# One head's scores as an fp32r product of stacked half terms, in the later batches of an attention and MLP kernel

## The chip, the cores and the metric

The kernel runs on one core of a Trainium2 chip. The metric is the device time of one execution in microseconds (us), from runs of the same program; lower is better.

## What is computed

The reference is a gated linear attention followed by a two-stage MLP. Cut to what matters:

```python
# q, k, v, o_gate: (4, 8, 768, 40); i_gate, f_gate: (4, 8, 768), all fp32
for t in range(S):
    m_new = maximum(f_gate[:, :, t] + m, i_gate[:, :, t])
    f_stab = exp(f_gate[:, :, t] + m - m_new); i_stab = exp(i_gate[:, :, t] - m_new); m = m_new
    C = f_stab * C + i_stab * outer(v_t, k_t)        # per batch and head, 40 x 40
    n = f_stab * n + i_stab * k_t
    y[:, :, t] = sigmoid(o_t) * (C @ q_t) / max(|n . q_t|, 1)
x = y as (4, 768, 320)
u = x + (relu(x.T @ w_tok1) @ w_tok2).T              # over the 768 tokens
out = u + relu(u @ w_ch1) @ w_ch2                    # over the 320 channels, 1536 hidden
```

## The kernel before

Time is cut into six chunks of 128 tokens. Within a chunk the recurrence becomes products: for each head the 128x128 scores k·q are multiplied by a matrix of decays and then applied to the values; the state of the chunks before enters by one more product. The eight heads go in three groups of 3, 3 and 2 heads (`HEADS`), so that a batch has 6 x 3 = 18 steps (`STEPS`). Step m belongs to chunk c = m // 3 and group g = m % 3. The program is written out by hand, one in-order list for each engine, with semaphores between them; nothing is scheduled by a planner.

**Where the attention of a batch runs.** Batch 0 has nothing beside it. The attention of batch b + 1 is spread over the MLP of batch b: its last stage has 24 slots (`SLOTS`), and in each slot every engine also does one place of `attention(b + 1, m)`. In batch 0 slot s holds place s - 3, in batches 1 and 2 slot s holds place s + 2, and places 0 and 1 stand in the stages before (`step_in`). A slot of the MLP is `hidden(slot)`, eight fp32r products of 384 columns on TensorE (lines 1222 to 1227); then `Relu` into `h_hi` on ScalarE (L755) and the remainder `h_lo` on VectorE (L974); then `project(slot)`, nine fp32r products of 320 columns (L1151). TensorE's order is hidden(s), the attention's place, project(s - 1).

**One place of the attention, for batches 1 to 3.** In the order of each engine:
- TensorE: the scores of step m (`step_scores`, L1063) into the one bank `pS`; the state's product (L1075); the values of step m - 2 (L1099, L1120).
- VectorE: `scores` (L851, `pS` times the decays in `gb`, which sets `p_ready`), `state` (L881, L890), `p_low` (L860), and in the places with g = 1 the five operations of `values` (L901 to L912).
- ScalarE: three exponentials of the next step (`exps`, L613), `p_high` (L623, waits for `p_ready`), in the places with g = 2 also `chunk_start` (L595, L599) and `x_high` (L647), in those with g = 0 `v_middle` (L603). With g = 2 the exponentials stand behind `p_high`.
- GpSimd: `rest` (L489, L491), `mask` (L499), and once a chunk `weigh` (L517), L551, L556, `scale_q` (L507) and `x_low` (L521).

**The score product.** The keys of a group, 3 heads x 40 rows, are the stationary operand `kd` (120 rows, 128 columns). The queries are in `qz`, in which each head has 128 columns of its own and zeros in the rows of the other heads, so that one fp32 product of 384 columns (256 in group 2) gives the scores of all heads of the group. `qz` is zeroed once, and three DMAs for each chunk fill the rows that are not zero.

**What the DMA queue does.** Nearly all loads stand in one list on SyncE. In it `load_chunk` for a chunk is `load_scores` (`kd`, `qz`), `load_decays` (`gb`), `load_values` (`kv`), `load_inter` (`gq`, `qd`). The two chunks (1, 0) and (1, 1) are followed by `load_o(1)`, the output gates of batch 1 into `x`, for which `sigmoid` on ScalarE waits in slot 1 of batch 0 (slot 0 in later batches). A wait in this list holds all that stands behind it.

## Time and profile before

| | us |
|---|---|
| median of 3 runs | 459.25 (458.14 to 460.07) |
| the profiled execution's own time | 460.83 |
| its span in the profile | 459.1 |
| TensorE busy | 440.7 (96%) |
| VectorE busy | 259.1 (56%) |
| ScalarE busy | 209.4 (46%) |
| GpSimd busy | 209.1 (46%) |
| chain that ended last, TensorE's share | 83% |

The profile is of one execution. A busy share is an average over stages with different limits, so that a change in one stage is judged by that stage's own rows. Names are PE for TensorE (PEld its weight loads), DVE for VectorE, ACT for ScalarE, POOL for GpSimd, SP for SyncE. Records of one engine overlap at their ends: the time that one operation takes from its engine is the distance from its start to the next start, a little less than its duration. An fp32 product shows as two records.

### The profile page before, as it was taken

Reading aid. Unit: us, or ns where it says so; the run is one execution under the profiler, and the core shown is the slowest. Engines: PE = TensorE matmul, PEld = TensorE weight load, DVE = VectorE, ACT = ScalarE, POOL = GpSimd, SP = SyncE. Lnnn points to the kernel's source line nnn. Section 1 sums busy time; section 2 is a strip of 40 time slices with the busy share of each in tenths; the row PEclk is TensorE's granted clock in tenths of the full one; section 3 lists DMA queues with packets and bytes.
Section 4 is the critical chain, followed back from the end, with each engine's and each line's share of the span. In section 5 each row is a group of like instructions: output and inputs, shape, how many; then the busy total and the mean of one; then the engine's idle time right before and its main releaser. Section 6 shows DMA issues by size and latency. Waiting matters only on the chain.

```text
span 459.1 us, 9511 instructions
## 1 busy us (share of the span) xinstructions
PE 440.7 (96%) x3463; PEld 407.9 (89%) x3463; DVE 259.1 (56%) x592; ACT 209.4 (46%) x517; POOL 209.1 (46%) x293
## 2 busy tenths in 40 slices
PE   7899989998999998999999998999999998999996
PEld 3587878998999997999999997899999997999996
DVE  8588965678865346776663236677674326222212
ACT  3665449665555247655552136755552213211120
POOL 7524410888886242988871204698883000000000
PEclk9899999999999999999999999999999999999999
DMA  7666991343344414544344013444410010000101
GB/s 215 191 172 192 348 256 39 104 115 129 95 134 136 140 44 115 148 127 131 127 152 141 1 44 87 144 135 140 126 60 1 1 43 1 0 2 0 45 1 43
DMA packets 36617, 47.38 MB, mean 103 GB/s; under 512 B 3357, under 2 KB 29083, under 8 KB 36571
## 3 DMA queue, kind: packets, MB, share of 16 engines
q1 hardware_dynamic: 35674, 45.76, 33.1%
q10 hardware_dynamic: 896, 1.02, 0.6%
q8 instruction: 28, 0.46, 0.4%
q14 instruction: 19, 0.15, 0.1%
HBM read 42.73 MB, written 4.03 MB: 102 GB/s over the span
## 4 chain that ended last, share of the span: by engine, by line
PE 83%; issue 6%; DVE 4%; ACT 3%; POOL 2%; DMA 1%; ACTq 0%; DVEq 0%; POOLq 0%
PE pC L1151 32%; PE pA L1222 7%; PE pA L1223 7%; PE pA L1224 7%; PE pS L1063 6%; PE pA L1151 5%; PE pY L1120 4%; PE pA L1226 3%; PE pA L1227 3%; PE pY L1099 2%; PE pN L1075 2%; DMA x<-o_gate_dram 1%; PE pA L1181 1%; POOL vw L517 1%; DVE pb L860 1%
## 5 line engine op out<-in xcount | busy, mean ns | idle before, releaser
L974 DVE SCALAR_TENSOR_TENSOR h_lo<-pA,h_hi 128x384 fp32r<-128x384 f32 x96 | 53.5, 557 | 148.0 <-ACT h_hi L755 147.9
L755 ACT ACTIVATE h_hi<-pA 128x384 fp32r<-128x384 f32 x96 | 46.9, 489 | 138.7 <-PE pA L1227 138.6
L1151 PE MATMUL pC<-wc_hi,h_hi 128*128 128x320 f32 x288 | 94.1, 327 | 0.8 <-DVE wc_lo L841 0.8
L1151 PE MATMUL pC<-wc_lo,h_hi 128*128 128x320 f32 x288 | 88.7, 308 | 0.0
L1151 PE MATMUL pC<-wc_hi,h_lo 128*128 128x320 f32 x288 | 88.5, 307 | 0.0
L489 POOL TENSOR_TENSOR gb<-gb,pb 128x384 f32<-128x384 f32 (+1 forms) x54 | 51.7, 957 | 65.7 <-ACT pb L623 65.4
L1222 PE MATMUL pA<-uT_hi,wc_hi 128*128 128x384 f32 x192 | 65.3, 340 | 1.9 <-DVE uT_hi L952 1.9
L1223 PE MATMUL pA<-uT_lo,wc_hi 128*128 128x384 f32 x192 | 64.7, 337 | 0.0
L1224 PE MATMUL pA<-uT_hi,wc_lo 128*128 128x384 f32 x192 | 64.3, 335 | 0.0
L1151 PEld LDWEIGHTS pC<-wc_hi,h_hi 128*128 128x128 f32 x288 | 54.0, 188 | 2.1 <-DVE h_lo L974 1.1
L1151 PEld LDWEIGHTS pC<-wc_lo,h_hi 128*128 128x128 f32 x288 | 54.2, 188 | 0.1
L1151 PEld LDWEIGHTS pC<-wc_hi,h_lo 128*128 128x128 f32 x288 | 54.0, 188 | 0.0
L613 ACT ACTIVATE gb<-gb,aT 128x128 f32<-128x128 f32 x144 | 47.6, 392 | 1.5 <-POOL gb L499 1.5
L1063 PE MATMUL pS<-qz,kd 120*128 120x384 f32 (+1 forms) x126 | 47.1, 454 | 0.0
L623 ACT ACTIVATE pb<-gb 128x384 bf16<-128x384 f32 (+1 forms) x54 | 26.4, 489 | 36.0 <-DVE gb L851 35.5
L860 DVE TENSOR_TENSOR pb<-gb,pb 128x384 bf16<-128x384 f32 (+1 forms) x54 | 38.6, 716 | 0.1
L1222 PEld LDWEIGHTS pA<-uT_hi,wc_hi 128*128 128x128 f32 x192 | 36.0, 187 | 3.0 <-DVE uT_hi L952 2.9
L521 POOL TENSOR_TENSOR x_lo<-x,x_hi 128x320 fp32r<-128x320 f32 x24 | 21.5, 896 | 33.4 <-ACT x_hi L647 33.4
L1224 PEld LDWEIGHTS pA<-uT_hi,wc_lo 128*128 128x128 f32 x192 | 36.0, 188 | 0.0
L1223 PEld LDWEIGHTS pA<-uT_lo,wc_hi 128*128 128x128 f32 x192 | 36.0, 188 | 0.0
L499 POOL TENSOR_SCALAR_AFFINE_SELECT gb<-gb 128x384 f32<-128x384 f32 (+1 forms) x54 | 29.8, 581 | 5.9 <-DMA gb<-g_dram 5.9
L851 DVE TENSOR_TENSOR gb<-pS,gb 128x384 f32<-128x384 f32 (+1 forms) x63 | 31.8, 504 | 1.1 <-PE pS L1063 0.8
(128 smaller groups left out, 885.0 us busy)
## 6 DMA issues: line engine op xcount, KB each, us to landing
gb<-g_dram SPq DMA_DIRECT2D x18, 512.0 KB, 4.0
kv<-kvN_dram SPq DMA_DIRECT2D x24, 324.0 KB, 4.1
kd<-kT_dram SPq DMA_DIRECT2D x24, 180.0 KB
qz<-qT_dram SPq DMA_DIRECT2D x72, 60.0 KB
out_dram<-u SPq DMA_DIRECT2D x24, 160.0 KB, 1.9
qd<-qT_dram SPq DMA_DIRECT2D x20, 180.0 KB, 2.6
gq<-g_dram SPq DMA_DIRECT2D x45, 60.0 KB
wc_raw<-w_ch_dram SPq DMA_DIRECT2D x6, 384.0 KB, 5.8
```

What stands on the lines that cost most here:

```text
L489: nc.gpsimd.tensor_tensor(tile, tile, pb[:, g, 0, 0:HEADS[g], :], ALU.subtract).then_inc(p_rest, 1)
L499: nc.gpsimd.affine_select(out=tile, in_=tile, compare_op=ALU.is_ge, fill=NEG, base=0, pattern=[[0, HEADS[g]], [1, L]], channel_multiplier= ...
L613: last = nc.scalar.activation(tile, tile, ACT.Exp, bias=aT[:, c, bass.ds(head, 1)])
L755: nc.scalar.activation(h2[0][:, slot % 2], pA[slot % 2][:, 0:HALF], ACT.Relu).then_inc(h2_hi, 1)
L851: nc.vector.tensor_tensor(tile, scores_bank(ba, m)[:, 0:n * L].rearrange("p (h t) -> p h t", h=n), tile, ALU.mult).then_inc(p_ready, 1)
L860: nc.vector.tensor_tensor(pb[:, g, 2, 0:n, :], gb[:, c % Q, GH * g:GH * g + n, :], pb[:, g, 1, 0:n, :], ALU.subtract).then_inc(p_split, 1)
L974: nc.vector.scalar_tensor_tensor(h2[1][:, slot % 2], pA[slot % 2][:, 0:HALF], 0.0, h2[0][:, slot % 2].bitcast(F32), ALU.max, ALU.subtract) ...
L1063: mm(scores_bank(ba, m)[:, 0:n * L], kd[0:n * D, r, g, :], qz[0:n * D, r, g, 0:n, :].rearrange("p h t -> p (h t)"), start=True, stop=True) ...
L1151: ins = mm(dst, a[p], b[q], start=first and n == 0, stop=last and n == 2)
L1222: mm(dst, wc1[0][:, t, f], uh[:, t, cols], start=t == 0, stop=False)
L1223: mm(dst, wc1[0][:, t, f], ul[:, t, cols], start=False, stop=False)
L1224: mm(dst, wc1[1][:, t, f], uh[:, t, cols], start=False, stop=False)
```

## The change

Batch 0 keeps the product above. From batch 1 on each head has an fp32r product of 128 columns of its own, three (or two) in a step. Both operands have 120 rows in which the 40 dimensions stand three times: rows 0 to 39 pair the keys' high half with the queries' remainder, rows 64 to 103 the keys' remainder with the queries' high half, and the other 40 rows the two high halves. So one pass sums three terms. The host lays the rows out in a new array `kq`.

The halves are made on the chip for every step: a load of 120 rows x 768 values into `kq_raw`; a copy to fp32r of the whole tile into `kq_stack` (`step_high`, ScalarE); two subtractions over 40 rows x 384 on VectorE (`step_low`), one for the keys, one for the queries, each on its rows alone. They stand at the end of place m for step m + 1 (places 2 to 5), for both m + 1 and m + 2 in place 6, and for m + 2 later; the last places make the first three steps of the next batch. The first three steps of batch 1 are made by GpSimd (`prepare_first`). `gq` has two buffers in place of three for the later batches, and `load_values` stands ahead of `load_decays`.

```diff
+FIRST_PREPARED = 3
+PREPARES_AT = 2
+TWO_AT = 6
+K_LOW, Q_LOW = slice(64, 64 + D), slice(0, D)
...
+        def prepares(ba, m):
+            if m < PREPARES_AT:
+                return []
+            steps = [m + 1] if m < TWO_AT else [m + 1, m + 2] if m == TWO_AT else [m + 2]
+            n = STEPS + (FIRST_PREPARED if ba < B - 1 else 0)
+            return [later(ba, k) for k in steps if k < n and later(ba, k) >= FIRST_PREPARED]
...
+            def load_step(ba, m):
+                c, g = divmod(m, NG)
+                k = later(ba, m)
+                if k < NG:
+                    sp.wait_ge(s_mm, STEPS)
+                elif k < NG + FIRST_PREPARED:
+                    sp.wait_ge(kq_first, 2 * (k - NG + 1))
+                else:
+                    sp.wait_ge(kq_lo, 2 * (k - NG - FIRST_PREPARED + 1))
+                sp.dma_start(kq_raw[:, g], kq[ba - 1, c, :, g]).then_inc(kq_in[g], 16)
...
             def load_rest(ba, c):
-                if ba > 0:
-                    load_decays(ba, c)
                 load_values(ba, c)
+                load_decays(ba, c)
+                load_step(ba, NG * c + 2)
                 if c > 0:
-                    load_inter(ba, c)
+                    load_query_decays(ba, c)
+                    load_queries(ba, c)
             def load_chunk(ba, c):
-                load_scores(ba, c)
+                load_two_steps(ba, c)
                 load_rest(ba, c)
...
+            def prepare_first(m):
+                _, g = divmod(m, NG)
+                pool.wait_ge(kq_in[g], 16)
+                raw, stack = step_tiles(kq_raw, g), step_tiles(kq_stack, g)
+                nc.gpsimd.tensor_copy(kq_stack[:, g, :, 0:HEADS[g], :], kq_raw[:, g, :, 0:HEADS[g], :]).then_inc(kq_first_hi, 1)
+                pool.wait_ge(kq_first_hi, m + 1)
...
+                    if n == NC:
+                        for m in range(FIRST_PREPARED):
+                            prepare_first(m)
                     pool.wait_ge(v_hi, n - NC + 1)
...
                 if ba > 0 and m % NG == 0 and 0 <= m < STEPS:
                     v_middle(ba, m // NG)
+                for k in prepares(ba, m):
+                    step_high(k)
                 c = chunk_at(ba, m, 1)
                 if c is not None:
                     x_high(ba, c)
+            def step_high(k):
+                g = k % NG
+                act.wait_ge(kq_in[g], 16 * (k // NG + 1))
+                act.wait_ge(s_mm, STEPS + k - NG + 1)
+                nc.scalar.activation(kq_stack[:, g, :, 0:HEADS[g], :], kq_raw[:, g, :, 0:HEADS[g], :],
+                                     ACT.Copy).then_inc(kq_hi, 1)
...
+                if ba > 0:
+                    for k in prepares(ba, m):
+                        step_low(k)
                 c = chunk_at(ba, m, 0)
                 if c is not None and (ba > 0 or c > 0):
                     values(ba, c)
+            def step_low(k):
+                raw, stack = step_tiles(kq_raw, k % NG), step_tiles(kq_stack, k % NG)
+                dve.wait_ge(kq_hi, k - FIRST_PREPARED + 1)
+                nc.vector.tensor_tensor(stack[0][K_LOW], raw[0][K_LOW], stack[0][K_LOW].bitcast(F32),
+                                        ALU.subtract).then_inc(kq_lo, 1)
+                nc.vector.tensor_tensor(stack[1][Q_LOW], raw[1][Q_LOW], stack[1][Q_LOW].bitcast(F32),
+                                        ALU.subtract).then_inc(kq_lo, 1)
...
+                pe.wait_ge(p_ready, STEPS + k)
+                for j in range(HEADS[g]):
+                    last = mm(scores_bank(ba, m)[:, j * L:(j + 1) * L], kq_stack[:, g, 0, j, :], kq_stack[:, g, 1, j, :],
+                              start=True, stop=True)
+                last.then_inc(s_mm, 1)
```

How the lists of the engines change, at three places. First VectorE, from the values of a chunk (end of a place with g = 1) through the place with g = 2. Before:

```order
L909 RECIPROCAL den<-den 128x8 [waits y_den]
L912 TENSOR_TENSOR x<-x,den 128x320 [waits y_read,y_den]
L974 SCALAR_TENSOR_TENSOR h_lo<-pA,h_hi 128x384 [waits h2_hi]
L851 TENSOR_TENSOR gb<-pS,gb 128x256 [waits e_exp,s_mm]
L881 TENSOR_TENSOR stn<-pN,blocks 120x123 [waits st_added,y_mm,n_mm]
L890 SCALAR_TENSOR_TENSOR st<-st,gq,stn 120x123 [waits n_read,st_added,gq_exp]
L860 TENSOR_TENSOR pb<-gb,pb 128x384 [waits p_mid]
L974 SCALAR_TENSOR_TENSOR h_lo<-pA,h_hi 128x384 [waits h2_hi]
```

And now:

```order
L1006 RECIPROCAL den<-den 128x8 [waits y_den]
L1009 TENSOR_TENSOR x<-x,den 128x320 [waits y_read,y_den]
L1084 SCALAR_TENSOR_TENSOR h_lo<-pA,h_hi 128x384 [waits h2_hi]
L948 TENSOR_TENSOR gb<-pS,gb 128x256 [waits e_exp,s_mm]
L978 TENSOR_TENSOR stn<-pN,blocks 120x123 [waits st_added,y_mm,n_mm]
L987 SCALAR_TENSOR_TENSOR st<-st,gq,stn 120x123 [waits n_read,st_added,gq_exp]
L957 TENSOR_TENSOR pb<-gb,pb 128x384 [waits p_mid]
L1031 TENSOR_TENSOR kq_stack<-kq_raw,kq_stack 40x384 [waits kq_hi]
L1033 TENSOR_TENSOR kq_stack<-kq_raw,kq_stack 40x384
L1084 SCALAR_TENSOR_TENSOR h_lo<-pA,h_hi 128x384 [waits h2_hi]
```

Two subtractions, which wait for ScalarE's `kq_hi`, stand ahead of the next slot's `h_lo`. In the place with g = 1 they stand ahead of the values too. Second, ScalarE in a place with g = 2 and the one with g = 0 behind it, before and now:

```order
L595 ACTIVATE gq<-gq 120x384 [waits gq_in2]
L599 ACTIVATE vb<-kv 128x328 [waits y_mm,kv_in1]
L647 ACTIVATE x_hi<-x 128x320 [waits h1_mm,x_ready]
L755 ACTIVATE h_hi<-pA 128x384 [waits c2_mm,c1_mm]
L613 ACTIVATE gb<-gb,aT 128x128 [waits g_masked]
L613 ACTIVATE gb<-gb,aT 128x128 x2
L623 ACTIVATE pb<-gb 128x384 [waits y_mm,p_ready]
L603 ACTIVATE vb<-kv 128x328 [waits v_rest]
L755 ACTIVATE h_hi<-pA 128x384 [waits c2_mm,c1_mm]
```

```order
L686 ACTIVATE vb<-kv 128x328 [waits y_mm,kv_in1]
L736 ACTIVATE kq_stack<-kq_raw 120x768 [waits s_mm,kq_in1]
L744 ACTIVATE x_hi<-x 128x320 [waits h1_mm,x_ready]
L852 ACTIVATE h_hi<-pA 128x384 [waits c2_mm,c1_mm]
L700 ACTIVATE gb<-gb,aT 128x128 [waits g_masked]
L700 ACTIVATE gb<-gb,aT 128x128 x2
L710 ACTIVATE pb<-gb 128x384 [waits y_mm,p_ready]
L690 ACTIVATE vb<-kv 128x328 [waits v_rest]
L736 ACTIVATE kq_stack<-kq_raw 120x2x256 [waits s_mm,kq_in2]
L852 ACTIVATE h_hi<-pA 128x384 [waits c2_mm,c1_mm]
```

The copy comes behind everything that its place had, apart from `x_hi`. Third, SyncE's list from chunk (1, 0) to the output gates of batch 1, before and now:

```order
L328 DMA gb<-g_dram 128x1024 [waits y_mm]
L341 DMA kv<-kvN_dram 128x648 [waits y_mm,n_mm]
L353 DMA gq<-g_dram 40x3x128 [waits st_added,q_scaled]
L353 DMA gq<-g_dram 40x3x128 x2
L357 DMA qd<-qT_dram 120x384 [waits y_mm]
L368 DMA x<-o_gate_dram 128x4x320 [waits u_ready]
```

```order
L369 DMA kq_raw<-kq_dram 120x768 [waits s_mm]
L369 DMA kq_raw<-kq_dram 120x768 [waits kq_first] x2
L391 DMA kv<-kvN_dram 128x648 [waits y_mm,n_mm]
L378 DMA gb<-g_dram 128x1024 [waits y_mm]
L369 DMA kq_raw<-kq_dram 120x768 [waits kq_first]
L405 DMA gq<-g_dram 40x3x128 [waits st_added,q_scaled]
L405 DMA gq<-g_dram 40x3x128 x2
L414 DMA qd<-qT_dram 120x384 [waits y_mm]
L425 DMA x<-o_gate_dram 128x4x320 [waits u_ready]
```

The load of the output gates now stands behind three loads that wait for `kq_first`, which GpSimd sets.

## Rows read from the trace of the kernel before

**Rows 1.** One chunk: us; busy us of PE, PEld, DVE, ACT, POOL; clock, DMA.

```profile
207.31:219.87 12.56, 12.56 (x119) 11.90 (x119) 8.43 (x20) 7.16 (x20) 10.48 (x14) 1.00 0.40 129
```

**Rows 2.** The chain of work that ended last, 203 to 216 us: start, us, what.

```profile
203.33 0.43 PE pS L1063 x2
...
207.47 0.65 PE pS L1063 x2
```

**Rows 3.** Timeline of TensorE, 36 to 40 us: start, us, instructions and their count.

```profile
35.94 0.33 PE L1032 MATMUL pA<-gp,pick 96*128 96x128 bf16 x3
36.11 0.42 PE L1075 MATMUL pN<-vw,kv 128*120 128x123 f32 x2
...
38.35 0.76 PE L1110 MATMUL pC<-kv,gb 128*128 128x41 f32 x6
38.95 0.89 PE L1063 MATMUL pS<-qz,kd 120*128 120x384 f32 x2
```

**Rows 4.** Timeline of ScalarE, 203 to 216.5 us; in brackets idle time before and releaser.

```profile
205.23 0.42 ACT L623 ACTIVATE pb<-gb 128x256 bf16<-128x256 f32 x1 [1.38 <-DVE gb L851]
...
207.22 0.46 ACT L647 ACTIVATE x_hi<-x 128x320 fp32r<-128x320 f32 x1
...
209.14 0.53 ACT L623 ACTIVATE pb<-gb 128x384 bf16<-128x384 f32 x1 [0.21 <-DVE gb L851]
210.25 0.48 ACT L603 ACTIVATE vb<-kv 128x328 bf16<-128x328 f32 x1 [0.58 <-POOL kv L551]
...
213.38 0.53 ACT L623 ACTIVATE pb<-gb 128x384 bf16<-128x384 f32 x1 [0.51 <-DVE gb L851]
```

**Rows 5.** Timeline of VectorE, the same stretch.

```profile
204.32 0.55 DVE L974 SCALAR_TENSOR_TENSOR h_lo<-pA,h_hi 128x384 fp32r<-128x384 f32 x1
...
205.80 1.04 DVE L860 TENSOR_TENSOR pb<-gb,pb 128x384 bf16<-128x384 f32 x1
208.09 0.56 DVE L974 SCALAR_TENSOR_TENSOR h_lo<-pA,h_hi 128x384 fp32r<-128x384 f32 x1 [1.25 <-ACT h_hi L755]
...
212.33 0.56 DVE L974 SCALAR_TENSOR_TENSOR h_lo<-pA,h_hi 128x384 fp32r<-128x384 f32 x1 [1.68 <-ACT h_hi L755]
...
213.95 0.55 DVE L860 TENSOR_TENSOR pb<-gb,pb 128x384 bf16<-128x384 f32 x1
214.42 0.49 DVE L901 TENSOR_TENSOR x<-pY,x 128x320 f32<-128x320 f32 x1
...
216.47 0.56 DVE L974 SCALAR_TENSOR_TENSOR h_lo<-pA,h_hi 128x384 fp32r<-128x384 f32 x1 [0.27 <-ACT h_hi L755]
```

**Rows 6.** Timeline of GpSimd, the same stretch.

```profile
205.74 0.69 POOL L489 TENSOR_TENSOR gb<-gb,pb 128x256 f32<-128x256 f32 x1 [1.07 <-ACT pb L623]
...
213.99 1.30 POOL L489 TENSOR_TENSOR gb<-gb,pb 128x384 f32<-128x384 f32 x1 [0.26 <-ACT pb L623]
```

**Rows 7.** Groups by line and shape: busy us, mean ns; then L489's ns, min/median/max.

```profile
L588 ACT ACTIVATE wc_hi<-wc_raw 128x768 fp32r<-128x768 f32 x6 | 4.9, 835 | 0.0
L491 POOL CAST pb<-gb 128x384 bf16<-128x384 f32 x36 | 19.4, 539 | 2.3
L489 POOL TENSOR_TENSOR gb<-gb,pb x54: 669/922/1301, 80.5 to 349.3; 128x384 f32<-128x384 f32 x36, 128x256 f32<-128x256 f32 x18
```

**Rows 8.** Timelines of GpSimd, SyncE and ScalarE in batch 0, 61 to 73 us.

```profile
61.58 1.37 POOL L499 TENSOR_SCALAR_AFFINE_SELECT gb<-gb 128x384 f32<-128x384 f32 x3 [5.91 <-DMA gb<-g_dram]
62.91 0.74 POOL L517 TENSOR_TENSOR vw<-kv,wT 128x328 f32<-128x328 f32 x1
...
63.45 3.13 SPq L368 DMA_DIRECT2D x<-o_gate_dram  x2
...
71.80 1.28 ACT L575 ACT_TABLE_LOAD   x1 [0.31 <-DMA x<-o_gate_dram]
```

**Rows 9.** Timelines of TensorE and ScalarE in slots 0 and 1 of batch 1.

```profile
182.01 0.81 PE L1063 MATMUL pS<-qz,kd 120*128 120x384 f32 x2
...
183.14 0.40 ACT L623 ACTIVATE pb<-gb 128x256 bf16<-128x256 f32 x1
```

More of the change, by code:

```diff
@@ L79, in step_in, with program @@
     return slot - BEHIND if b == 0 else slot + AHEAD
-def program(nc, qT, kT, kvN, i_gate, f_gate, o_gate, w_tok1, w_tok2, w_ch1, w_ch2, out):
+def program(nc, qT, kT, kq, kvN, i_gate, f_gate, o_gate, w_tok1, w_tok2, w_ch1, w_ch2, out):
     ctx = ExitStack()
@@ L163, in program, with gq_at, step_tiles @@
         pN = bank("pN")
+        def gq_at(ba, c):
+            if ba == 0:
+                return gq_first[:, :, :] if c % Q == R else gq[:, c % Q]
+            return gq[:, c % R]
+        def step_tiles(tensor, g):
+            return [tensor[:, g, side, 0:HEADS[g], :] for side in range(2)]
         def scores_bank(ba, m):
@@ L179, in program @@
         gb_in = [sem(f"gb_in{i}") for i in range(Q)]
-        gq_in = [sem(f"gq_in{i}") for i in range(Q)]
+        gq_in = [sem(f"gq_in{i}") for i in range(R)]
+        kq_in = [sem(f"kq_in{i}") for i in range(NG)]
+        kq_hi = sem("kq_hi")
+        kq_lo = sem("kq_lo")
+        kq_first_hi = sem("kq_first_hi")
+        kq_first = sem("kq_first")
         g_out = sem("g_out")
@@ L1125, in attention @@
             def attention(ba, m):
-                if m < STEPS:
+                if m < STEPS and ba > 0:
                     step_scores(ba, m)
                 if ba == 0:
+                    if m < STEPS:
+                        first_scores(m)
                     if m in (1, 4):
@@ L1265, in rows, with stacked @@
         return np.ascontiguousarray(padded.reshape(B, NG, ROWS, NC, L).transpose(0, 3, 2, 1, 4))
+    def stacked(a):
+        order = np.r_[0:D, 0:64 - D, 0:D, 64 - D:D]
+        heads = np.concatenate([a[1:], np.zeros((B - 1, NG * GH - H, S, D), np.float32)], axis=1)
+        return heads.reshape(B - 1, NG, GH, NC, L, D).transpose(0, 3, 5, 1, 2, 4)[:, :, order]
     def by_partition(w, k):
```

133 lines of the change are left out of this document (82 added, 51 removed).

## The prediction

> **What bounds the kernel now.** I read first one chunk of the attention of batch 2 beside the MLP of batch 1, three slots [rows 1]: TensorE is busy for all of its 12.56 us at full clock, VectorE for 8.43, ScalarE for 7.16, GpSimd for 10.48. The chain that ended last runs through nothing but TensorE there, and the score products are links of it, 0.65 us in groups of three heads and 0.43 in the group of two [rows 2]. So a shorter product is a gain, for as long as TensorE is still what ends last. I then read the three helpers, since the change pays for the product with work on them. VectorE's idle time before `h_lo` is 1.25, 1.68 and 0.27 us in the three slots [rows 5], 3.20 a chunk: it is the nearest to its limit, above all in the slot with the values. GpSimd's idle time is 2.08. What the work beside TensorE waits for in turn is in the ScalarE rows [rows 4]: `p_high` starts 1.05 us after `h_lo` (209.14 against 208.09, 213.38 against 212.33; 0.91 for two heads), and `v_middle` starts when GpSimd's chain behind `x_hi` is through, 3.03 us later (207.22 to 210.25).
>
> **The product.** Batches 1 to 3 have 54 steps, 36 with three heads and 18 with two. No row shows an fp32r product of 128 columns. From below: a bf16 one with its weight load takes 0.057 us (three in 0.17) [rows 3]. From above: a third of the fp32 product, 0.217 [rows 2]. Nearest is the small product of L1110, whose time is that of loading 128 columns of 4-byte weights: six in 0.60 us, 0.10 each [rows 3]. I take 0.11. A step then takes 0.33 in place of 0.65 or 0.22 in place of 0.43: TensorE is relieved of 36 x 0.32 + 18 x 0.21 = 15.3 us, 0.85 a chunk. Ends: 22.9 with 0.057, and 0 with 0.217.
>
> **The work that is added,** a chunk: three copies on ScalarE of 768, 768 and 512 values, the first two at 0.84 us each by the weights' copy [rows 7], the last at 0.60, between that and the 0.53 of 384 values [rows 4]; and six subtractions on VectorE, four of 384 values and two of 256. A VectorE operation of 384 takes 0.47 from start to start (213.95 to 214.42) [rows 5], so 0.94 for a pair, 0.68 for the pair of 256. By sum alone they would almost fit: VectorE's 9.36 us of occupied time and 2.56 new make 11.92, TensorE's chunk would be 11.71.
>
> **Where they stand decides.** Within a slot VectorE does `h_lo` and the scores, ScalarE waits for them with `p_high`, then copies; VectorE waits for the copy with its pair, and only then comes to the next slot's `h_lo`. That is a ring through both engines, which TensorE's slack can't shorten. From one `h_lo` to the next:
> - place with g = 2: 0.91 to `p_high`, 1.99 for it, the three exponentials and `chunk_start` (205.23 to 207.22), copy 0.84, pair 0.94: 4.68.
> - place with g = 0: `x_hi` now starts 3.74 after the former `h_lo`, `v_middle` 3.03 later, at 6.77 [rows 4]; with its 0.48, the copy of 0.60 and the pair of 0.68 it is 8.53, so this place takes 3.85.
> - place with g = 1: 1.05, `p_high` 0.53, copy 0.84, pair 0.94, then the values, 214.42 to 216.47 less 0.27 idle, 1.78: 5.14.
>
> The ring is 13.67 a chunk, more than TensorE's old 12.56. To it comes what VectorE and GpSimd take from each other. A VectorE operation with both inputs in SBUF that meets a GpSimd one is longer by 0.49 (L860 at 205.80, 1.04 against 0.55, behind L489 at 205.74), and in the other order GpSimd's is longer by 0.38 (1.30 against its median 0.92) [rows 5 to 7]. Each added subtraction is such an operation, and GpSimd is busy for 0.83 of a chunk. For a random meeting I take 0.25 each, 1.5 a chunk; the ends are 0 and 0.49. I so take 15.2 a chunk, against 12.56: 2.64 more. The Trainium skill (SBUF — State Buffer, Who interferes with whom) has this as a rule that speaks against the change: a VectorE instruction with two SBUF inputs and a GpSimd one that reads SBUF exclude each other, and the second waits for the whole of the first. The rows agree. By that rule alone a meeting could cost a whole GpSimd operation, 0.92 of L489, and the chunk up to 13.67 + 6 x 0.92 = 19.2, a time near 565; the rows' two meetings cost half of that or less.
>
> From place 2 to place 17 there are five chunks in each of three batches: 15 x 2.64 = **+39.6**. The product's 15.3 us are not to be taken off, since in these chunks TensorE waits; the six steps in places 0 and 1 stand among waits and I count them at nothing (at most 1.9 off). At the start of each batch VectorE may fall behind for a while before TensorE notices: scores that TensorE began at 207.47 [rows 2] are out of `pS` at 209.1, a 0.47 and a 0.55 behind `h_lo` at 208.09 [rows 5], and the next product comes a slot of 4.2 us later, at 211.7; some 2.5 us are free, three times: **-7.5**.
>
> **The queue in batch 0.** The gates of batch 1 were issued from 63.45 to 66.58 us and ScalarE, which had waited 0.31, found them at 71.80: 5.2 us from issue, and no slack [rows 8]. Now they stand behind loads that wait for `prepare_first`. GpSimd's `mask` began at 61.58, when `gb` had landed, and `weigh` ended at 63.65 [rows 8]; 360 KB more are ahead of `gb`, by the shapes, some 1.1 us at the 129 / 0.40 = 322 GB/s of all queues' time [rows 1]. Then come three steps, each a copy, near 1.0 at twice the 0.54 of 384 values, and two subtractions of 0.92 [rows 7]: 2.84, 2.84 and for two heads 2.0, until 72.4. The load of step 5, three of `gq` and `qd` take SyncE to 74.6, the gates themselves to 74.9, and they land at 80.1: **+8.3**. Nothing covers it, since the next slot's `h_hi` stands behind the sigmoid. Ends: 4, with a preparation half as long, and 11.
>
> **Slot 0 of batches 1 and 2.** The sigmoid and its table loads hold `p_high` until 183.14 there, while the next product began at 182.01 [rows 9]. Step 3 is made only one place ahead: `p_high` 0.40, copy 0.84, pair 0.94, so its product can't begin before 185.3. That is 3.3 later, less 0.3 for the shorter product, twice: **+6.0**.
>
> **Sum.** 39.6 - 7.5 + 8.3 + 6.0 = 46.4. The profiled execution took 460.8, so 507.2; the median of the runs lies 1.6 below it. **Forecast 506 us**, 10% slower. By their shapes the loads grow from 1556 to 2276 KB a chunk, at a DMA share of 0.40 [rows 1]: to about 0.6, which I cost at nothing while a step's buffer is loaded some three slots, 12 us, ahead of its copy; without that cover each microsecond late goes into the ring.
>
> **Rivals.**
> 1. *The ring without collisions.* If the subtractions seldom meet GpSimd's operations, the chunk is 13.67: 15 x 1.11 + 6.8 = 23.5, so 483. For it: they come later than `p_low`, which now meets L489 most. Against: GpSimd is busy for 0.83 of the chunk.
> 2. *Every subtraction meets one at the full 0.49:* 13.67 + 2.94 = 16.6 a chunk, 15 x 4.05 + 6.8 = 67.6, so 527. GpSimd's delays would make `v_middle` late as well, which is in the ring. The Trainium skill's rule on the two engines, named above, would send it this way.
> 3. *Faster.* The ring doesn't close, because the copy is ready by the time VectorE is through with `p_low`, and `h_lo` needn't be early: TensorE asks for it only after the next hidden stage. Then the sum of VectorE's work bounds, 11.92 a chunk: 15 x -0.64 = -9.6, and if the queue's stall is hidden, 450; with the stall 458, no change. It decides at the copy's end: ScalarE would have to end it within some 2.6 us of `h_lo` (208.09 to the end of `p_low`) in all three places. By the rows it is 3.74, 7.85 - 4.68 = 3.17 and 2.42, so only the third holds.
> 4. *The product is no shorter,* at 0.217 a head. Then TensorE's chunk stays at 12.56, and the ring decides as before: 506 again. It would show only in the product's rows; only where the ring doesn't close is it a time of its own, 467.5 with the queue's stall.
>
> **Chances.** Forecast, with or without rival 4: 0.60. Rival 1: 0.18. Rival 2: 0.12. Rival 3: 0.06 faster and 0.02 the same, and 0.02 for anything that just cancels. What a measurement of this kernel can tell from no change is about 0.5%, 2.3 us. That gives 0.06 faster, 0.04 the same, 0.90 slower. The range reaches over rivals 1 and 2: 478 to 528. What it leaves out is the faster side with cases below the first rival, and above it long waits of TensorE in which its clock falls.
>
> **What would show it.** Fp32r products of 128 columns starting 0.10 to 0.12 us apart. VectorE idle ahead of the first subtraction with ScalarE's `kq_stack` as the releaser, in the places with g = 0 and 2 above all. A chunk of 15 us in the middle of each batch, TensorE waiting there for `h_lo` or for the subtractions. L489 and the subtractions longer when they meet. One wait of TensorE near 77 us of about 8 us, with the sigmoid of batch 1 starting near 80. In slots 0 of later batches a product that waits 3 us for VectorE. The forecast is wrong if VectorE's subtractions start without waiting, if TensorE is busy for over 95% of a chunk, or if the chunk stays under 13 us: then sums of work are the bound, and the product's rows tell rival 3 from 4.

## The result, and the profile after

The changed kernel takes **540.97 us**, the median of 4 runs (540.37 to 541.38), against 459.66 (458.14 to 460.37) for the kernel before beside it: ratio 1.177, 95% interval 1.174 to 1.181. The forecast was 506 with 478 to 528: the sign was right, and the size too small by 35 us. The profiled execution's span is 539.1 us.

The profile page of the changed kernel, TensorE's line and the row of its granted clock over the span in 40 slices, and two lines of its summary of the chain that ended last:

```profile
PE 453.9 (84%) x3499; PEld 427.2 (79%) x3499; DVE 323.9 (60%) x694; ACT 241.8 (45%) x568; POOL 232.5 (43%) x302
PEclk9899995888989899989989999987979899999999
PE 51%; DVE 16%; issue 11%; ACT 9%; DMA 7%; POOL 5%; SPq 1%; DVEq 0%; ACTq 0%; POOLq 0%
```

TensorE's share of the chain fell from 83% to 51%, and its clock shows dips that it had not. Six rows out of the view of waits, of TensorE and of its helpers (us in total, times, longest):

```profile
DVE kq_stack L1031 <- ACT kq_stack L736: 42.8, 39, 5.2
PE pS L1187 <- DVE kq_stack L1033: 25.7, 9, 5.8
PE pY L1223 <- DVE x L998: 21.7, 10, 3.3
POOL gb L567 <- DMA gb<-g_dram: 21.6, 7, 9.8
ACT L660 <- DMA x<-o_gate_dram: 15.6, 1, 15.6
PE pC L1277 <- DVE h_lo L1084: 13.7, 1, 13.7
```

The first is the ring that was forecast. The second and the fourth are the ones that the forecast had not, nor had it the third: TensorE waits there, behind the state's product, for VectorE to take the former values out of `pY` into `x`. A fifth wait of TensorE is new, for `u`, a sum of the MLP on VectorE: 7.6 us in three places.

All nine waits in the second row lie at the products of places 3 to 6. From place 7 on no product waits for its subtractions.

**The product** did what it says. TensorE's timeline, a group of three heads, one of two and the row behind each:

```profile
227.27 0.55 PE L1187 MATMUL pS<-kq_stack 120*128 120x128 f32 x3 [1.12 <-DVE kq_stack L1033]
227.66 0.42 PE L1199 MATMUL pN<-vw,kv 128*120 128x123 f32 x2
...
231.33 0.44 PE L1187 MATMUL pS<-kq_stack 120*128 120x128 f32 x2
231.60 0.42 PE L1199 MATMUL pN<-vw,kv 128*120 128x123 f32 x2
```

0.39 and 0.27 us, 0.13 a head, where the fp32 product took 0.65 and 0.43 [rows 2].

**The chunk.** The attention of batch 2 beside the MLP of batch 1: the chunk from place 6 to 9, the one from 9 to 12 (its window ends 0.16 us behind the start of the product, 273.30), and the one from 7 to 10, whose products wait for no load (columns as in [rows 1]):

```profile
241.56:256.55 14.99, 13.49 (x119) 13.27 (x120) 12.43 (x26) 6.88 (x16) 10.48 (x13) 0.89 0.67 180
256.55:273.46 16.91, 13.65 (x123) 13.46 (x122) 13.30 (x28) 9.92 (x24) 11.69 (x15) 0.90 0.49 140
247.09:260.52 13.43, 11.94 (x120) 11.76 (x120) 11.15 (x24) 7.61 (x19) 8.24 (x11) 1.00 0.68 177
```

**Where the 81 us arose.** I took the start of every score product of batches 1 to 3 in both timelines of TensorE and subtracted. The lag grows like this; the forecast's column puts its own terms on the same stretches (2.64 us a chunk, 0.88 a place, less 2.5 at each start):

| stretch | forecast | batch 1, 2, 3 | sum |
|---|---|---|---|
| up to place 2 of batch 1 | 8.3 | 14.4 | 14.4 |
| place 2 to 3 | 8.6 | 3.4, 3.6, 3.6 | 10.6 |
| place 3 to 6 | 0.4 | 6.9, 6.7, 5.3 | 18.9 |
| place 6 to 15 | 23.8 | 7.2, 7.8, 9.4 | 24.3 |
| place 15 to place 2 of the next batch, or to the last | 5.3 | 4.6, 3.4, 3.6 | 11.7 |
| together | 46.4 | | 79.9 |

The nine chunks between places 6 and 15 cost 2.70 us each, where the forecast had 2.64. Of the miss of 33.5 us in this profile 18.5 stand in places 3 to 6, 6.4 behind place 15, 6.1 in the stall of batch 0 and 2.0 in place 2. Behind place 15 TensorE waits for the `x` of the last chunk (3.0 and 1.5 us at the ends of batches 1 and 2) and for `u` (2.5 and 2.6 us in batches 2 and 3), both VectorE's.

**Waiting, and slower work.** The same 81 us divided another way. The kernel with the product alone (below) has as many instructions on TensorE as the changed one, 3499, and a granted clock of 1.00; this is its row of busy times:

```profile
PE 427.8 (94%) x3499; PEld 404.7 (89%) x3499; DVE 271.2 (60%) x592; ACT 209.0 (46%) x517; POOL 217.0 (48%) x302
```

Its span is 453.6 us. The changed kernel's is 85.5 longer: TensorE is idle for 59.4 us more (85.2 against 25.8), and busy for 26.1 us more (453.9 against 427.8) with the same number of instructions, at a mean granted clock of 0.936.

**The stall of batch 0.** SyncE, GpSimd and ScalarE there, each from its timeline, to be read beside [rows 8]:

```profile
51.33 22.75 SPq L369 DMA_DIRECT2D kq_raw<-kq_dram  x3
...
78.41 0.96 SPq L425 DMA_DIRECT2D x<-o_gate_dram  x2
```

```profile
64.49 1.36 POOL L567 TENSOR_SCALAR_AFFINE_SELECT gb<-gb 128x384 f32<-128x384 f32 x3 [9.76 <-DMA gb<-g_dram]
...
66.62 0.83 POOL L576 CAST kq_stack<-kq_raw 120x768 fp32r<-120x768 f32 x1
...
75.29 0.72 POOL L580 TENSOR_TENSOR kq_stack<-kq_raw,kq_stack 40x256 fp32r<-40x256 f32 x1
```

```profile
86.13 1.28 ACT L660 ACT_TABLE_LOAD   x1 [15.57 <-DMA x<-o_gate_dram]
```

`mask` began at 64.49, not 62.7: `gb` came 2.9 us later than before, not 1.1. The forecast counted 360 KB more ahead of it; by the lists of the change it is 684, two steps' loads of 360 and the values' 324 in place of the 360 of `kd` and `qz`, which would be 2.1 us at the forecast's rate. The three steps took until 76.0, 9.4 us for 7.7. The gates were issued from 78.41 (forecast 74.9 for their end) and landed 6.8 us behind the end of their issue, not 5.2. So the sigmoid began at 86.13, 14.3 us later than before; the forecast had 8.3.

### The profile page after: what moved, and what is told of

The parts are those of the page before. It is cut to its first block, busy times and chain, and to the rows that moved or that the text cites. A ratio compares the mean times of both kernels' runs of the same rounds, so it can differ in the third digit from the quotient of the medians.

```text
span 539.1 us, 9818 instructions
## 1 busy us (share of the span) xinstructions
PE 453.9 (84%) x3499; PEld 427.2 (79%) x3499; DVE 323.9 (60%) x694; ACT 241.8 (45%) x568; POOL 232.5 (43%) x302
## 2 busy tenths in 40 slices
DMA packets 34456, 60.65 MB, mean 112 GB/s; under 512 B 3356, under 2 KB 20442, under 8 KB 34410
## 4 chain that ended last, share of the span: by engine, by line
PE 51%; DVE 16%; issue 11%; ACT 9%; DMA 7%; POOL 5%; SPq 1%; DVEq 0%; ACTq 0%; POOLq 0%
PE pC L1277 21%; PE pA L1348 4%; PE pA L1349 4%; DMA gb<-g_dram 4%; PE pA L1350 4%; DVE kq_stack L1033 3%; PE pA L1277 3%; ACT kq_stack L736 3%; DVE gb L948 2%; DVE kq_stack L1031 2%; PE pC L1111 2%; PE pA L1353 2%; PE pA L1352 2%; PE pY L1244 2%; DVE h_lo L1084 2%
## 5 line engine op out<-in xcount | busy, mean ns | idle before, releaser
L1277 PE MATMUL pC<-wc_hi,h_hi 128*128 128x320 f32 x288 | 99.3, 345 | 22.2 <-DVE h_lo L1084 13.7
L1277 PE MATMUL pC<-wc_hi,h_lo 128*128 128x320 f32 x288 | 93.5, 325 | 0.0
L1277 PE MATMUL pC<-wc_lo,h_hi 128*128 128x320 f32 x288 | 93.4, 324 | 0.0
L1277 PEld LDWEIGHTS pC<-wc_hi,h_hi 128*128 128x128 f32 x288 | 57.8, 201 | 23.7 <-DVE h_lo L1084 14.9
L1031 DVE TENSOR_TENSOR kq_stack<-kq_raw,kq_stack 40x384 fp32r<-40x384 f32 (+1 forms) x51 | 35.2, 690 | 43.1 <-ACT kq_stack L736 42.8
L1277 PEld LDWEIGHTS pC<-wc_lo,h_hi 128*128 128x128 f32 x288 | 58.3, 202 | 0.0
L1277 PEld LDWEIGHTS pC<-wc_hi,h_lo 128*128 128x128 f32 x288 | 58.0, 201 | 0.0
L1187 PEld LDWEIGHTS pS<-kq_stack 120*128 120x128 f32 x144 | 24.5, 203 | 29.1 <-DVE kq_stack L1033 29.1
L1187 PE MATMUL pS<-kq_stack 120*128 120x128 f32 x144 | 24.8, 277 | 25.9 <-DVE kq_stack L1033 25.7
L1033 DVE TENSOR_TENSOR kq_stack<-kq_raw,kq_stack 40x384 fp32r<-40x384 f32 (+1 forms) x51 | 41.8, 820 | 1.6
L1223 PE MATMUL pY<-st,qd 120*128 120x123 f32 (+1 forms) x102 | 21.8, 297 | 21.7 <-DVE x L998 21.7
```

The costliest lines, as they stand in the source:

```text
L1031: nc.vector.tensor_tensor(stack[0][K_LOW], raw[0][K_LOW], stack[0][K_LOW].bitcast(F32), ALU.subtract).then_inc(kq_lo, 1)
L1033: nc.vector.tensor_tensor(stack[1][Q_LOW], raw[1][Q_LOW], stack[1][Q_LOW].bitcast(F32), ALU.subtract).then_inc(kq_lo, 1)
L1187: last = mm(scores_bank(ba, m)[:, j * L:(j + 1) * L], kq_stack[:, g, 0, j, :], kq_stack[:, g, 1, j, :], start=True, stop=True)
L1277: ins = mm(dst, a[p], b[q], start=first and n == 0, stop=last and n == 2)
```

## The experiments

All edits are made to the changed kernel, whose 541.0 us is meant where a gain is told. Most were run two times only, and two such runs of one kernel lie up to 6 us apart. Lags are those of the table.

**The stall alone.** The gates of batch 1 are issued from ScalarE's queue, ahead of `attention(1, -1)`:

```diff
-                    load_o(b + 1)
+                    if b > 0:
+                        load_o(b + 1)
...
                 if b == 0:
+                    next_o = o_gate[1, :, :].rearrange("(c p) d -> p c d", p=L)
+                    for i, (first, last) in enumerate(O_PARTS):
+                        act.dma_start(x[:, first:last], next_o[:, first:last]).then_inc(o_in[i], 16)
                     attention(1, -1)
```

> The output gates of batch 1 are issued from ScalarE's queue, after the last transposed tile of batch 0, in place of SyncE's list; nothing else moves. Theory (the list holds the gates back, and the stall goes straight to the end): TensorE's wait of 14 us in slot 1 of batch 0 goes, the sigmoid starts near 72 instead of 86, the time falls by 12 to 15 us from 541 to 527. Rival (the first product of batch 1 waits for GpSimd's preparation anyway, which ends at 76): the wait only moves on, and the time falls by 4 us or less.

522.88 us (520.6 to 525.2), ratio 1.137. 18.1 us are back, and the lag at place 1 of batch 1 is -1.8 where it was 14.7: shown. By the lag the stall is 16.5 us there; the two runs lie 4.6 us apart, so that the rest of the 18.1 may be nothing.

**The product alone.** From the fourth step on nothing is loaded, copied or subtracted; every product reads again the operands of one of the first three steps, so the scores are those of other data:

```diff
-            n = STEPS + (FIRST_PREPARED if ba < B - 1 else 0)
+            n = 0
...
+                if k >= NG:
+                    return
                 if k < NG:
                     sp.wait_ge(s_mm, STEPS)
...
-                else:
-                    pe.wait_ge(kq_lo, 2 * (k - FIRST_PREPARED + 1))
```

> The new products stay, but only the first three steps' operands are loaded and split; from the fourth step of batch 1 on the products read those three again (so the scores of all later steps are those of the first three), and there are no loads, copies or subtractions for them. Theory (the product is cheaper by 0.33 us a step, and only its preparation costs): TensorE ends last in every chunk, a chunk takes 11.7 us instead of 12.56, the time is 443 to 450. Rival (the short product is no shorter than the fp32 one): 456 to 462.

457.65 us (455.5 to 459.3), ratio 0.9964 (0.9944 to 0.9985). The gain is 1.6 us, a tenth of the 15.3 that the forecast gave the shorter products. The theory (443 to 450) missed; the time is the rival's, but not its reason, since the product is shorter. TensorE's timeline of a group of three and the slot with the values:

```profile
204.36 0.45 PE L1187 MATMUL pS<-kq_stack 120*128 120x128 f32 x3
204.65 0.32 PE L1199 MATMUL pN<-vw,kv 128*80 128x82 f32 x2
...
212.15 0.34 PE L1187 MATMUL pS<-kq_stack 120*128 120x128 f32 x2
212.32 0.42 PE L1199 MATMUL pN<-vw,kv 128*120 128x123 f32 x2
213.15 0.46 PE L1223 MATMUL pY<-st,qd 120*128 120x123 f32 x2 [0.41 <-DVE x L1000]
```

and its chunk, one row of windows:

```profile
199.80:212.15 12.35, 11.93 (x121) 11.75 (x121) 9.47 (x21) 6.80 (x18) 10.35 (x15) 1.00 0.32 101
```

The products take 0.29, 0.29 and 0.17 us, 0.98 a chunk less than before. The chunk is 12.35 us, 0.21 less. In the slot behind the values TensorE comes to `pY` before VectorE's `x` has emptied it, and 0.83 us pass between two products that stood 0.21 apart before (216.19 and 216.40 in the trace of before). So 0.62 of the 0.98 us go there: before the change VectorE was already late enough, once a chunk, to take nearly two thirds of what a faster TensorE gains.

**Loads, copies, subtractions.** Three kernels add the work back one kind at a time: the loads of all steps without copies and subtractions (the products read old operands); loads and copies without subtractions (the remainders are left out); and subtractions over 12 of the 128 columns of a head (the rest of the remainders is left out). What a load waits for differs with them: for the former product and load in the first, for the copy in the second. The products of all three give other scores, as with the product alone.

> The loads of every step stay; from the fourth step of batch 1 on the copies and the subtractions are left out, and the products wait for the load and read the operands of the first three steps. Theory (the loads cost only the stall of batch 0 and some late decays): 541 less the subtractions' 46 and less 8 to 15 for the copies, 480 to 487; nearly all of it above 446 is the stall of 14 us and waits for gb. Rival (the copies cost nothing, the loads carry the rest): 492 or more.

> VectorE's subtractions are left out (the products then read operands without their remainders, so part of the scores is missing); the product and the next load wait for the copy instead. Theory (the ring and the collisions are VectorE's subtractions): the time falls by 30 to 50 us, to 491 to 511, and GpSimd's busy time falls by 5 us or more. Rival (the loads and ScalarE's copies are the cause): under 15 us.

```diff
-        nc.vector.tensor_tensor(stack[0][K_LOW], raw[0][K_LOW], ...
+        nc.vector.tensor_tensor(stack[0][K_LOW, :, 0:12], raw[0][K_LOW, :, 0:12], ...
```

> All of VectorE's subtractions stay at their places with their waits, but each takes 12 columns of every head, 36 or 24 in place of 384 or 256 (the rest of the remainders isn't made). Theory (the ring is made of waits, which stay, and of 0.35 to 0.9 us of work and collisions, which go): each pair is shorter by 1.1 to 1.4 us, a half to two thirds of the 46 us of leaving them out: 508 to 518. Rival A (all is in their length and in the collisions): 495 to 500. Rival B (all is in the order of waits): 530 or more.

| kernel | us | added by it |
|---|---|---|
| product alone | 457.65 | |
| and the loads | 474.79 | 17.1 |
| and the copies | 494.5 | 19.7 |
| and the subtractions, 12 columns | 516.42 | 21.9 |
| and their whole width | 540.97 | 24.6 |

The shares hold for this order of adding. The loads' 17 us are the stall of batch 0: against the product alone the lag is 17.3 more at place 1 of batch 1 and 19.6 at the end. Loads that wait for nothing of the ring cost little more, 2 us at most, although they move as many bytes as those of the changed kernel (60.65 MB). Half of what the subtractions cost is their width, that is VectorE's time and its meetings with GpSimd; the other half comes with two instructions and their waits, whatever their width.

**The ring.** The copy stands first in ScalarE's place, ahead of the exponentials, so that it is done before VectorE comes to the subtractions:

```diff
             def attention(ba, m):
+                for k in prepares(ba, m):
+                    step_high(k)
                 if 0 <= m + 1 < STEPS and (m + 1) % NG:
                     exps(ba, m + 1)
...
-                for k in prepares(ba, m):
-                    step_high(k)
```

> ScalarE makes its copy of a step's operands first in its place, ahead of the exponentials and of p_high, so that it doesn't stand behind the scores of the same place. Theory (ring): VectorE's 43 us of waiting ahead of its first subtraction fall below 10, and the time falls by 12 to 30 us, to 511 to 529. Rival (VectorE and GpSimd are bound by the added work and by each other): the wait goes, but turns up ahead of other operations, and the time falls by under 8 us.

523.44 us (521.3 to 525.6), 17.5 less. VectorE's wait for the copy falls from 42.8 us in 39 places to this row:

```profile
DVE kq_stack L1031 <- ACT kq_stack L736: 4.6, 2, 2.3
```

But where did the gain arise? Between places 3 and 6 the lag grows by 7.5 us in place of 18.9, and behind place 15 by 3.9 in place of 11.7. In the nine chunks between, for which the ring had been worked out, nothing is won: 25.4 us for 24.3. The sums of windows over these nine chunks (from the product of place 6 to that of place 15 in each batch), of before, of the changed kernel and with the copy first:

```profile
sum 114.61, PE 113.39 PEld 107.28 DVE 83.18 ACT 64.87 POOL 95.43; mean PE 37.80 PEld 35.76 DVE 27.73 ACT 21.62 POOL 31.81
sum 138.93, PE 119.34 PEld 117.64 DVE 113.08 ACT 73.61 POOL 98.60; mean PE 39.78 PEld 39.21 DVE 37.69 ACT 24.54 POOL 32.87
sum 139.98, PE 117.45 PEld 114.33 DVE 121.47 ACT 80.77 POOL 100.75; mean PE 39.15 PEld 38.11 DVE 40.49 ACT 26.92 POOL 33.58
```

VectorE is busy for 121.5 us in place of 113.1 with the same operations: what it no longer waits it spends in longer ones. TensorE waits in these chunks for `x`, 17.1 us in the changed kernel and 17.5 with the copy first.

The other way to open the ring, the subtractions one place behind their copy:

```diff
-PREPARES_AT = 2
-TWO_AT = 6
+PREPARES_AT = 1
+TWO_AT = 0
...
-                    for k in prepares(ba, m):
+                    for k in prepares(ba, m - 1):
                         step_low(k)
```

> Each pair of subtractions stands one place behind its copy, at the end of the next place, and every step is copied two places ahead. Theory: VectorE then never waits for the copy, the ring through ScalarE is open, and what is left is VectorE's own work: the gain of copying first (17.5 us) or more, 515 to 525, with no row in which L1031 waits for L736. Rival, the product now asks for its pair in the very next place, and the raw tile is given back a place later, so that the loads behind it on SyncE's queue come later still: 540 to 560.

532.11 us (529.2 to 535.0), between the theory and the rival: the wait for the copy is gone from the list of waits, but TensorE's wait for the subtractions is 47.0 us in 31 places, and GpSimd waits 41.5 us for `gb`. The slack that the copy won was paid by the product.

**One place ahead.** In places 2 to 5 of the changed kernel a step is copied and subtracted in the place just before its product, and place 6 does two. The chain of waits of batch 2 there, a stretch without TensorE:

```profile
216.74 0.96 ACT L660
...
219.75 0.40 ACT pb L710
220.15 0.73 ACT kq_stack L736
...
224.34 0.75 ACT kq_stack L736
...
225.10 0.84 DVE kq_stack L1031
...
225.98 1.25 DVE kq_stack L1033
```

The product at 227.27 waits for the last of these. The edit is one number, `TWO_AT = 2` in place of 6: place 2 makes steps 3 and 4, and each later place is two ahead.

> TWO_AT is 2 in place of 6: place 2 makes steps 3 and 4, and from place 3 on each step is made two places ahead. Theory: in places 2 to 5 a step is made one place ahead, so TensorE waits there for the whole of copy and subtractions, 6.2, 5.1 and 4.6 us from product to product where 4.0 was before; with two places ahead the waits of places 4 to 6 go, at the price of one longer place 2: 2 to 4 us a batch, 541 less 6 to 12, so 529 to 535. Rival, VectorE's and ScalarE's ring is full in these places too, and the double place costs the same wherever it stands: 539 to 543.

521.96 us (521.5 to 522.4), 19.0 less, more than the theory gave. The lag grows by 3.1, 1.7 and 1.7 us from place 3 to 6, in place of 6.9, 6.7 and 5.3, 12.3 us of the gain; another 5.4 come behind place 15, none in the nine chunks between (24.2 us for 24.3). TensorE's wait for the subtractions falls from 25.7 to 10.4 us, in three places.

**The loads' order.** The chain above goes on like this (SPq is SyncE's queue):

```profile
227.24 0.35 SPq L369
...
228.09 8.50 DMA gb<-g_dram
...
239.05 0.74 ACT kq_stack L736
...
239.82 0.56 DVE kq_stack L1031
...
241.56 0.92 PE pS L1187 x3
```

A step's load waits for the subtraction that frees its tile; the decays of the next chunk stand behind it, land 8.5 us later (4.0 is the median before), GpSimd's mask and ScalarE's exponentials wait for them, and the next copy stands behind these. The distance to this product is 10.2 us. Three edits were made against it. First, the decays ahead of the two step loads of their chunk:

```diff
             def load_two_steps(ba, c):
+                load_decays(ba, c)
                 load_step(ba, NG * c)
...
                 load_values(ba, c)
-                load_decays(ba, c)
```

> In SyncE's list the load of the decays stands first in its chunk again, ahead of the loads of the steps and of the values. Theory (late decays lengthen the ring: mask, exponentials, copy, subtractions all stand behind them): the seven waits of GpSimd's mask for gb, 21.6 us in all, fall below 8, and the time falls by 10 to 18 us. Rival (the ring of copy and subtractions bounds without them): mask waits less, but the time falls by under 4 us.

540.1 us (539.8 to 540.5): nothing, as the rival had it. In its chain the query decays, issued behind the same step loads, had taken the place:

```profile
224.71 0.62 DVE kq_stack L1033
...
225.35 0.32 SPq L369
...
226.50 4.05 DMA gq<-g_dram
...
231.37 0.83 ACT kq_stack L736
```

Second, from chunk 2 on the decays, the values and the query decays all ahead of the steps:

```diff
+                load_decays(ba, c)
+                load_values(ba, c)
+                load_query_decays(ba, c)
+                load_two_steps(ba, c)
+                load_step(ba, NG * c + 2)
+                load_queries(ba, c)
```

> From chunk 2 of each later batch on, SyncE issues the decays, the values and the query decays of a chunk ahead of its three step loads, not behind two of them. Theory: the changed kernel has a second ring, from a subtraction over SyncE's step load, the decays or query decays issued behind it, GpSimd's mask and ScalarE's exponentials back to the copy and the next subtraction; moving the decays alone (540.1) only passed the place on to the query decays. With all of them ahead no wait for gb, gq or kv is left in places 5 and 11, the distance from product 5 to product 6 falls from 8.2, 10.2 and 8.1 us to about 6, and 11 to 12 from 8.9 and 10.0 to about 5.5: 541 less 12 to 22, so 519 to 529. Rival, the ring of VectorE and ScalarE alone sets the time and catches up whatever the loads give back: 536 to 541, as with the decays alone.

534.86 us (534.8 to 534.9), 6.1 less and not 12 to 22. The distance from the product of place 5 to that of 6 fell from 8.2, 10.2 and 8.1 to 7.7, 6.9 and 6.9 us, and not to 6; from 11 to 12, where 5.5 was expected in batches 2 and 3, it went from 8.9 and 10.0 to 9.7 and 9.8. Now the raw tiles were late, in the chain again:

```profile
257.54 3.94 DMA kq_raw<-kq_dram
...
261.50 0.85 ACT kq_stack L744
```

Third, the step loads on ScalarE's queue, behind `p_high`, where no load of SyncE stands behind them:

```diff
                     p_high(ba, m)
+                if ba > 0:
+                    for k in prepares(ba, m - 1):
+                        load_after(k)
...
+            def load_after(k):
+                act.wait_ge(kq_lo, 2 * (k - FIRST_PREPARED + 1))
+                k = k + NG
```

> The changed kernel with only the step loads moved to ScalarE's queue, behind p_high. Theory: 10 to 22 us less, 519 to 531, more than the 6 us that the other order of SyncE's list gave, since here neither kind of load waits behind the other. Rival: 0.35 us of issue in each place goes into the ring and takes the gain away, 536 to 550.

533.94 us (533.9 to 534.0), 7.0 less, between the theory and the rival. Two unlike cures give the same, so 6 to 7 us of the late loads can be had back. That they cost no more isn't shown, since each cure has a price of its own: late raw tiles in the one, 0.35 us of ScalarE for each issue in the other. From place 6 to 15 the lag grows by 27.5 and 27.3 us with them, no less than without.

**Together.** Four kernels with several edits: gates, decays first and copy first; gates, all loads ahead, two steps at place 2 and copy first; gates, two steps and copy first; and these three with the step loads on ScalarE's queue.

> Gates from ScalarE's queue, decays first in their chunk, and the copy first in its place: the edits of the first three runs together. Theory (the stall of batch 0 and the ring are separate costs that add up): 523 - 18 = 505, and less if the early decays count once the ring is open: 500 to 507. Rival (they hide each other): 515 or more.

> Four edits together: the gates of batch 1 on ScalarE's queue, decays, values and query decays ahead of the step loads, two steps at place 2, the copy at the start of its place. Theory: they remove different waits, so their gains add: 541 less 18, 17.5, 12 to 22 and 6 to 12 is 471 to 487; a floor is the kernel with copies but no subtractions less its stall, 494.5 less 18, 476, plus what the subtractions take from GpSimd by collisions, so 480 to 492. Rival, only one wait at a time sets the pace and the others catch up: 500 to 506, the time of the three edits already run together.

> Three edits: the gates of batch 1 on ScalarE's queue (alone 18 us), two steps at place 2 (alone 19), the copy first in its place (alone 17.5); the order of SyncE's list is the changed kernel's. Theory: the order of that list only decides which load is late (6 us alone, and then the raw tiles were late), so without it the four-edit kernel's 495.4 is reached or passed: 541 less 54.5 is 486.5, so 484 to 492. Rival, the loads' order was part of what the four edits gave: 498 to 505.

> The three edits and the step loads issued by ScalarE behind p_high, so that no load of decays, values or queries stands behind one that waits for a subtraction. Theory: the late loads are the rest of the second ring; 8 to 18 us below the kernel with the three edits, so 470 to 480, with no wait of GpSimd for gb or of ScalarE for kq_raw over 2 us in the middle of a batch. Rival, ScalarE is in the ring and each issue holds it 0.35 us, 54 of them 19 us: no gain over the three edits, 486 to 500.

505.85 us (504.1 to 507.6), as expected; 495.42 (494.5 to 497.0) and 496.59 (496.1 to 498.5), 15 and 10 us above the sums of their parts, and outside of what theory or rival gave for either; and 499.46 (497.3 to 499.8), the rival. The gains add until something else is the bound. In the kernel with three edits the nine chunks between places 6 and 15 at last cost less, 14.8 us in place of 24.3, and over a whole chunk VectorE's timeline has no wait for another engine; some of its rows:

```profile
221.62 0.47 DVE L1002 TENSOR_TENSOR x<-pY,x 128x320 f32<-128x320 f32 x1
...
225.59 0.64 DVE L1035 TENSOR_TENSOR kq_stack<-kq_raw,kq_stack 40x384 fp32r<-40x384 f32 x1
226.26 0.55 DVE L1037 TENSOR_TENSOR kq_stack<-kq_raw,kq_stack 40x384 fp32r<-40x384 f32 x1
...
228.78 0.93 DVE L1035 TENSOR_TENSOR kq_stack<-kq_raw,kq_stack 40x256 fp32r<-40x256 f32 x1
229.74 1.03 DVE L1037 TENSOR_TENSOR kq_stack<-kq_raw,kq_stack 40x256 fp32r<-40x256 f32 x1
...
234.25 0.74 DVE L1035 TENSOR_TENSOR kq_stack<-kq_raw,kq_stack 40x384 fp32r<-40x384 f32 x1
235.02 0.76 DVE L1037 TENSOR_TENSOR kq_stack<-kq_raw,kq_stack 40x384 fp32r<-40x384 f32 x1
235.71 0.47 DVE L1002 TENSOR_TENSOR x<-pY,x 128x320 f32<-128x320 f32 x1
```

From `x` to `x` it is 14.09 us, against TensorE's 12.56 before and 12.35 with the product alone. VectorE is busy for 13.37 of it, and the rest are steps of under 0.2 us from one operation to the next. What GpSimd's operations lengthen is within these times. The six subtractions take 4.65. So with the edits that gained most together the change is still a loss of 8% here, and no version beat the kernel before but the one that doesn't prepare its operands, by 0.4%. Not every wait was removed: TensorE still waits 6.4 us for subtractions in the kernel with three edits.

## Why the prediction was right and wrong

- **The sign: right. The ring: right as a wait, wrong as what bounds the middle of a batch.** "VectorE waits for the copy with its pair, and only then comes to the next slot's `h_lo`" is the first of the waits shown, 42.8 us, and copying first gave 17.5 back. The nine chunks between places 6 and 15 lie 2.70 us above those of before, forecast 2.64. That agreement is luck in good part. With the copy first, the wait for it is nearly gone, and these chunks cost 25.4 us as before that edit 24.3. With subtractions over 12 columns, and the ring's waits left as they are, they cost 15.0, with none 8.2. So most of their cost is VectorE's work, and TensorE meets it at `x`, not at `h_lo` or at the subtractions, as the forecast's signs had it. The nine are between 13.2 and 17.8 us long, and the two shortest, 13.15 and 13.75, lie about the 13.67 of the ring without collisions; the long ones hold late loads, waits for `x` and `u`, and slow stretches of TensorE.
- **The collisions: right in size.** L1031 and L1033 with 384 values take 695 and 909 ns in the mean where a free one takes 0.55 us: 0.25 each, the number used. The Trainium skill's rule (SBUF — State Buffer, Who interferes with whom) was the reason to look; by its bound, a whole GpSimd operation for each meeting, the time would have been 565, and the means above are a quarter of that. Other operations of VectorE did not get longer: `p_low` with 384 values takes 788 ns in the mean for 852 before, the product of `x` and `den` 524 for 613. It may be that the new operations took over meetings of the old ones; that isn't shown.
- **"At the start of each batch VectorE may fall behind for a while before TensorE notices ... -7.5": wrong, and the largest miss,** 18.5 us. The slack was read off a place in the middle, where the product is two places behind its operands. From place 2 to 5 it is one place behind, and TensorE notices at once: its nine waits for the subtractions, 25.7 us, are all there. With the steps two ahead 19.0 us came back, 12.3 of them in places 3 to 6 by the lag.
- **"I cost at nothing" the loads' growth: wrong** by at least the 6 to 7 us that two unlike experiments gave back. The tile was indeed loaded ahead of its copy. What was late stood behind that load in SyncE's list. The text named the condition, but not who waits in the queue.
- **The stall of batch 0: right in kind, 8.3 for 14.3.** Its four terms were each too small: landing of `gb` 1.1 for 2.9, the three steps 7.7 for 9.4, the queue from there to the gates' issue 2.5 for 3.4, the gates' flight 5.2 for 6.8. The first is in the main a miscount of what stands ahead of `gb`. Undone, the stall gave 18.1, 16.5 of it by the lag at place 1. TensorE comes out of its wait of 13.7 us at a lower clock, 0.53 granted from 90.2 to 95.1 us, and that is part of the 16.5.
- **The sigmoid's slot: right in size,** 3.6 from place 2 to 3 for 3.0 and the 0.88 of any place. But batch 1 loses 3.4 there with no sigmoid in its slot: ScalarE does the copy of a weight, three exponentials and `chunk_start` ahead of the copy, and the product waits 3.1 us for the subtractions all the same. So the one place of distance costs this much with other work in the way too, and that was left out.
- **Behind place 15: 11.7 for 5.3,** with the waits for the last `x` and for `u` told above. No term of the sum had them, and no experiment was made for them alone.
- **The product: right in the row, wrong in what it is worth.** 0.09 to 0.13 us a head for 0.11. "The product's 15.3 us are not to be taken off" held. But rival 3 took TensorE's chunk without the ring as 11.71; with nothing added at all it is 12.35, since VectorE's `x` is next in line. And VectorE's sum, put at 11.92, is 14.09 in a chunk in which it never waits. So the faster case had some 3 us to win from TensorE, 0.21 in each of 15 chunks, and VectorE's work stood against it.
- **The clock was left out.** The projection of a slot, nine products, in the chain behind a wait and in the next slot:

```profile
269.22 2.58 PE pC L1277 x9
...
274.61 1.41 PE pC L1277 x9
```

  By TensorE's timeline 12 of the 88 groups of nine are longer by over 0.15 us than the median of 1.40 after the change, 1 before, and they hold 10.8 us of lengthening against 0.2. But the projections are less than half of it: over all its instructions TensorE is busy for 26.1 us more than with the product alone, at granted clocks of 0.936 and 1.00. Eleven of the 12 groups begin at most 2.2 us behind the end of a wait of TensorE of 2.4 to 13.7 us, the first of the two above behind one of 3.3: there, for all or part of the group, the clock is at the lower of its two levels, 1.2 in place of 2.4 GHz. Three waits of 2.5 to 3.0 us have no such group behind them. Where VectorE ends last, a slower TensorE costs nothing. How much of the 26 lay on the chain was not separated. The sum has no term for it; the range named "long waits of TensorE in which its clock falls" among what it leaves out.

## What to carry to other kernels

A bound of 96% busy doesn't say what a shorter instruction is worth: look for the wait that is next, which here took nearly two thirds of it. When an account agrees with the measured chunk, open the wait that it names and look at that same chunk: here the gain came elsewhere. When work is put on a helper, price it at the place with the least distance to its consumer, not in the middle of the loop; and when a load is given a new condition, look at everything behind it in its queue. Before paying with a second engine's time, add up that engine's whole chunk with the lengthened rows: here 14.1 us of VectorE against 12.6 of TensorE are a loss by themselves.

## What was not expected of the hardware

Subtractions over 12 columns of a head instead of 128 still cost 21.9 us of the 46.5; one with 36 values takes 328 or 400 ns in the mean (its two lines), one with 384 takes 695 or 909. With its waits for the copy gone, VectorE was busy for 8.4 us more in nine chunks with the same operations. The fp32r product of 128 columns takes 0.29 us for three where nothing waits and 0.39 behind a wait. The decays' load of 512 KB, 4.0 us in the median before, took 5.9 after, and 8.5 in the chain, with three step loads, values and query decays issued within a few us of it; from 228 to 237 us, around that one, the DMA engines were busy for a share of 0.84, where a chunk has 0.5 to 0.7.
